# A three-stage attention and MLP kernel: splits, sums and loads of its last two stages put in another order

## The reference, cut to what matters

```python
attn = attention(q, k, v)                     # batch 4, 8 heads, 576 tokens, 64 wide; two window masks
xk = mu_k * x + (1 - mu_k) * x_prev           # x is attn as [4, 576, 512], x_prev is x one token back
xr = mu_r * x + (1 - mu_r) * x_prev
x = sigmoid(xr @ w_r) * (relu(xk @ w_k) ** 2 @ w_v)
h = relu(x.transpose(0, 2, 1) @ w_tok1) @ w_tok2      # over tokens: 576 -> 256 -> 576
u = x + h.transpose(0, 2, 1)
out = u + relu(u @ w_ch1) @ w_ch2                     # over channels: 512 -> 1536 -> 512
```

## Time and profile before

| | us |
|---|---|
| median of 3 runs | 744.74 |
| range of the runs | 740.33 to 745.08 |
| the profiled execution | 743.76 |
| its span in the profile | 741.9 |
| TensorE busy (matmul) | 672.7, 91% of the span |
| VectorE, ScalarE, GpSimd busy | 493.7, 320.2, 260.3 |

### The profile page before, as it was taken

How to read it: one execution, slowest core, us unless ns; L and a number is a source line. 1 busy time by engine, 2 the same in 40 slices (tenths; PEclk the granted TensorE clock), 3 DMA queues, 4 the chain that set the end, 5 groups by cost and what they waited for, 6 DMA issues and landing times.

```text
span 741.9 us, 17173 instructions
## 1 busy us (share of the span) xinstructions
PE 672.7 (91%) x6977; PEld 647.4 (87%) x6977; DVE 493.7 (67%) x836; ACT 320.2 (43%) x676; POOL 260.3 (35%) x289
## 2 busy tenths in 40 slices
PE   8999999999999999994898788999697639999997
PEld 7879999999999999993787788999697639989997
DVE  5588876766777676782476767767386336574855
ACT  4573645354444534541442255636264224142530
POOL 5575746464646464611863411120301300000000
PEclk9999999999999999998899979999898959999999
DMA  9962433324323316229671343546786494969783
GB/s 192 252 140 51 79 66 55 63 54 88 61 55 62 75 38 127 79 63 177 144 262 65 125 164 123 189 145 217 237 266 228 151 373 166 232 258 243 240 236 65
DMA packets 210174, 109.46 MB, mean 148 GB/s; under 512 B 163112, under 2 KB 199088, under 8 KB 209584
## 3 DMA queue, kind: packets, MB, share of 16 engines
q1 hardware_dynamic: 200144, 103.06, 50.1%
q10 hardware_dynamic: 9952, 5.31, 3.0%
HBM read 69.41 MB, written 38.93 MB: 146 GB/s over the span
## 4 chain that ended last, share of the span: by engine, by line
PE 68%; DMA 10%; DVE 9%; SPq 6%; ACT 2%; POOL 2%; issue 2%; POOLq 0%; DVEq 0%
PE bank L961 8%; PE bank L963 7%; PE bank L962 7%; PE tq L961 3%; DMA ck__raw<-h_rows 3%; SPq L1835 3%; PE tq L962 3%; PE tq L963 3%; PE bank L837 2%; DMA W__raw<-in_moe_w_ch 2%; PE bank L1556 2%; PE bank L1016 2%; PE bank L1558 2%; PE bank L1557 2%; PE s L625 2%; PE tq L1556 2%
## 5 line engine op out<-in xcount | busy, mean ns | idle before, releaser
L1744 ACT ACTIVATE ck__hi<-ck__raw 128x576 fp32r<-128x576 f32 x84 | 51.4, 674 | 85.3 <-DMA ck__raw<-h_rows 85.3
L1748 DVE TENSOR_TENSOR ck__lo<-ck__raw,ck__hi 128x576 fp32r<-128x576 f32 x84 | 58.9, 747 | 37.8 <-ACT ck__hi L1744 37.8
L1556 PE MATMUL bank<-U__hi,W__hi 128*128 128x288 f32 x192 | 59.8, 312 | 17.9 <-ACT hq L1592 11.9
L1056 POOL TENSOR_TENSOR k_lo<-kr,k_hi 128x288 fp32r<-128x288 f32 x64 | 56.2, 882 | 25.4 <-ACT k_hi L1052 25.4
L1098 DVE RECIPROCAL rg<-rg 128x288 f32<-128x288 f32 x32 | 61.4, 1922 | 0.0
L1557 PE MATMUL bank<-U__hi,W__lo 128*128 128x288 f32 x192 | 58.8, 306 | 0.0
L1558 PE MATMUL bank<-U__lo,W__hi 128*128 128x288 f32 x192 | 58.5, 305 | 0.0
L961 PE MATMUL bank<-k_hi,WV_hi 128*128 128x288 f32 x184 | 55.5, 301 | 0.0
L1556 PEld LDWEIGHTS bank<-U__hi,W__hi 128*128 128x128 f32 x192 | 38.1, 199 | 19.1 <-ACT hq L1592 12.4
L962 PE MATMUL bank<-k_hi,WV_lo 128*128 128x288 f32 x184 | 54.3, 295 | 0.0
L963 PE MATMUL bank<-k_lo,WV_hi 128*128 128x288 f32 x184 | 54.1, 294 | 0.0
(11 more groups left out here) (253 smaller groups left out, 2341.2 us busy)
## 6 DMA issues: line engine op xcount, KB each, us to landing
h_rows<-hq SPq DMA_DIRECT2D x24, 1008.0 KB, 4.6
ck__raw<-h_rows SPq DMA_DIRECT2D x28, 864.0 KB, 5.5
W__raw<-in_moe_w_ch SPq DMA_DIRECT2D x7, 768.0 KB, 7.9
x_turned<-xblocks SPq DMA_DIRECT2D x16, 288.0 KB, 5.2
u_kept<-X SPq DMA_DIRECT2D x4, 1152.0 KB, 8.8
ub<-u_kept SPq DMA_DIRECT2D x4, 1152.0 KB, 6.9
xT_raw<-x_turned SPq DMA_DIRECT2D x4, 1024.0 KB, 5.8
out_x<-ob SPq DMA_DIRECT2D x56, 72.0 KB, 3.4
```

The costliest lines, as they stand in the source:

```text
L1056: e.tensor_tensor(lo, t, hi.bitcast(F32), ALU.subtract).then_inc(Z.lo_done, 1)
L1556: e.matmul(ps, wh[:, w], xh[:, x], start=not onto and kt == 0, stop=False, skip_group_check=onto)
L1744: e.activation(hi, raw, ACT.Copy).then_inc(Z.ch_done, 1)
L1748: e.tensor_tensor(lo, raw, hi.bitcast(F32), ALU.subtract).then_inc(Z.cl_done, 1)
```

## The change

It touches the last three lists of steps, the places of some tiles and a few semaphores; the arithmetic is the same.

- `x_blocks(1)` goes three units earlier in `phase1`. `x_rows` is cut in `x_out` (store) and `x_in` (read back), placed apart; batch 3's blocks get a place of their own (that of batch 1's), so they no longer wait for batch 2's store.
- In the token stage `x_blocks(2)`, `x_blocks(3)` and the w1 sums come first, `token_up(b, 0)` goes ahead of `x_parts(b + 1)`, `token_up(b, 1)` behind it, and splits are moved.
- The sums are cut in single steps (`w1_sum`, `u_sum`, `w2_sum`). Those of w1 slice 2, of u for batches 2 and 3, and S1 and S2 of w2 go from GpSimd to VectorE.
- `u_parts` splits in the order in which TensorE uses the parts, and each half product waits for its own operand's split, not for all seven.
- `load_w2` has four parts, of which the first two come behind steps 7 and 11 (before: step 15). `w2_parts` for A12, S3, S4 and A22 come after the up stage's last step. `W2`, `CK`, `ub` and `ob` lie elsewhere, so that `load_h(2)` and `load_h(3)` can come behind step 22.

```diff
-        W2, o = [], 0
-        for i in range(7):
-            if i == 3:
-                o = R0
-            w, o = weights(f"W2_{i}_", [P, NJ * 2 * P], o)
-            W2.append(w)
-        a11_again = at("a11_again", [P, NJ * 2 * P], F32, R0 + 8 * NJ * 2 * P)
+        W2_AT = [0, 8 * NJ * 2 * P, 16 * NJ * 2 * P, R0, R0 + 8 * NJ * 2 * P, U1, U1 + 8 * NJ * 2 * P]
+        W2 = [weights(f"W2_{i}_", [P, NJ * 2 * P], off)[0] for i, off in enumerate(W2_AT)]
+        a22_first, a11_again = [at(n, [P, NJ * 2 * P], F32, W2_AT[i]) for n, i in (("a22_first", 1), ("a11_again", 4))]
+        NCK = 4
+        CK_AT = [U0, U0 + 8 * NJ * HALF, R0 + NSL1, R0 + NSL1 + 8 * NJ * HALF]
+        CK = [weights(f"ck{i}_", [P, NJ * HALF], off)[0] for i, off in enumerate(CK_AT)]
+        o = R0 + 2 * NSL1
         ub = [at(f"ub{i}", [P, DT * S], F32, o + 4 * DT * S * i) for i in range(2)]
-        o += 8 * DT * S
-        ob = at("ob", [P, DT * S], F32, o)
-        o += 4 * DT * S
-        NCK = 4
-        CK = [weights(f"ck{i}_", [P, NJ * HALF], (U0, U1)[i // 2] + 8 * NJ * HALF * (i % 2))[0] for i in range(NCK)]
-        assert o <= U0 and U0 + 16 * NJ * HALF <= U1 and U1 + 16 * NJ * HALF <= HQ0
+        ob = at("ob", [P, DT * S], F32, o + 8 * DT * S)
+        assert CK_AT[3] + 8 * NJ * HALF <= o and o + 12 * DT * S <= U0 and W2_AT[2] + 8 * NJ * 2 * P <= R0 - 4 * P - 16 * DT
...
-        xblocks = (xblocks0, xblocks1, xblocks2, xblocks2)
+        xblocks = (xblocks0, xblocks1, xblocks2, xblocks3)
...
+        def w1_sum(s, k):
             raw = [w[2][:, :] for w in W1[s]]
...
+            made, first = (Z.w1_last_sums, 0) if s == NSL - 1 else (Z.w1_sums, 4 * s)
+            def queue(e):
+                if k == 0:
+                    e.wait_ge(w1_in[s], 64)
+                    e.tensor_tensor(raw[S1], raw[S3], raw[A22], ALU.add).then_inc(made, 1)
+                elif k == 1:
+                    e.wait_ge(made, first + 1)
+                    e.tensor_tensor(raw[S2], raw[S1], raw[A11], ALU.subtract).then_inc(made, 1)
+                elif k == 2:
+                    e.wait_ge(made, first + 1)
+                    e.tensor_tensor(raw[S3], raw[A11], raw[S3], ALU.subtract).then_inc(made, 1)
+                else:
+                    e.wait_ge(made, first + 2)
+                    e.tensor_tensor(raw[S4], raw[A12], raw[S2], ALU.subtract).then_inc(made, 1)
+            return dict(vector=queue) if s == NSL - 1 else dict(gpsimd=queue)
...
-        U_ORDER = (B11, T1_, B21, B22, T3_, T2_, T4_)
+            def queue(e):
...
+            return dict(gpsimd=queue) if b < 2 else dict(vector=queue)
...
+                if j_ == 0:
+                    e.wait_ge(Z.ul_done, 7 * b_ + U_ORDER.index(i) + 1)
+                if b_ == 0 and j_ % 2 == 0:
+                    e.wait_ge(Z.w1_lo, 7 * (j_ // 2) + i + 1)
...
                 if part == 0:
                     e.wait_ge(Z.u_kept, 16 * B)
+                    e.wait_ge(Z.ul_done, 7 * 2)
+                    e.dma_start(tiles(W2[A11][2][:, :], NJ), w2_block(0, 0)).then_inc(Z.w2_in0, 16)
+                elif part == 1:
+                    e.wait_ge(Z.ul_done, 7 * 3)
+                    e.dma_start(tiles(W2[S1][2][:, :], NJ), w2_block(1, 0)).then_inc(Z.w2_in1, 16)
+                    e.dma_start(tiles(a22_first[:, :], NJ), w2_block(1, 1)).then_inc(Z.w2_in1, 16)
+                elif part == 2:
+                    e.wait_ge(Z.p4_done, NQ - 4)
+                    e.dma_start(tiles(W2[A12][2][:, :], NJ), w2_block(0, 1)).then_inc(Z.w2_in2, 16)
+                    e.dma_start(tiles(W2[S3][2][:, :], NJ), w2_block(1, 0)).then_inc(Z.w2_in2, 16)
+                    e.dma_start(tiles(a11_again[:, :], NJ), w2_block(0, 0)).then_inc(Z.w2_in2, 16)
+                else:
+                    e.wait_ge(Z.p4_done, NQ)
+                    e.dma_start(tiles(W2[S4][2][:, :], NJ), w2_block(0, 1)).then_inc(Z.w2_in3, 16)
+                    e.dma_start(tiles(W2[A22][2][:, :], NJ), w2_block(1, 1)).then_inc(Z.w2_in3, 16)
+            return dict(sync=sync)
...
+            def vector(e):
+                if i == S1:
+                    e.wait_ge(Z.w2_in1, 32)
+                    e.tensor_tensor(raw[S1], raw[S1], a22_first[:, :], ALU.add).then_inc(Z.w2_sums, 1)
+                else:
+                    e.wait_ge(Z.w2_in0, 16)
+                    e.wait_ge(Z.w2_sums, 1)
                     e.wait_ge(Z.ul_done, 7 * B)
...
+                    e.tensor_tensor(raw[S2], raw[S1], raw[A11], ALU.subtract).then_inc(Z.w2_sums, 1)
+            def gpsimd(e):
+                if i == S3:
+                    e.wait_ge(Z.w2_in2, 48)
+                    e.tensor_tensor(raw[S3], a11_again[:, :], raw[S3], ALU.subtract).then_inc(Z.w2_last_sums, 1)
                 else:
...
+                    e.wait_ge(Z.w2_in3, 32)
                     e.wait_ge(Z.w2_lo, S2 + 1)
...
+                    e.tensor_tensor(raw[S4], raw[S4], W2[S2][0][:, :].bitcast(F32), ALU.subtract).then_inc(Z.w2_last_sums, 1)
+                    e.wait_ge(Z.w2_last_sums, 2)
+                    e.tensor_tensor(raw[S4], raw[S4], W2[S2][1][:, :].bitcast(F32), ALU.subtract).then_inc(Z.w2_last_sums, 1)
+            return dict(vector=vector) if i in (S1, S2) else dict(gpsimd=gpsimd)
...
-                    e.wait_ge(Z.p4_done, NQ)
+                    e.wait_ge(Z.p4_done, NQ - 2)
...
-                ff[d // 2 - 6].append(x_blocks(1, d))
-            ff[-31].append(x_rows(0))
-            ff[-4].append(x_rows(1))
+                ff[d // 2 - 9].append(x_blocks(1, d))
+            ff[-31] += [x_out(0), x_in(0)]
+            ff[-7].append(x_out(1))
+            ff[-1].append(x_in(1))
...
-            steps = [x_parts(1, i) for i in range(NTT)] + [x_blocks(2, d) for d in range(DT)] + [x_rows(2)]
-            steps += [token_up(0, m) for m in range(2)] + [w1_sums(0)] + [x_parts(2, i) for i in range(NTT)]
-            steps += his(w1[0]) + token_rows(0) + [x_blocks(3, d) for d in range(DT)] + [x_rows(3), keep_u(0), u_sums(0)]
-            steps += [token_up(1, m) for m in range(2)] + his(u0) + [x_parts(3, i) for i in range(NTT)]
-            steps += los(w1[0])[:3] + token_rows(1) + [load_w1(1), keep_u(1)] + los(w1[0])[3:] + [w1_sums(1)]
-            steps += [token_up(2, m) for m in range(2)] + los(u0)[:3] + token_rows(2) + [keep_u(2)] + los(u0)[3:]
-            steps += [token_up(3, m) for m in range(2)] + his(w1[1]) + los(w1[1])[:3] + token_rows(3)
-            steps += [load_w1(2), keep_u(3), w1_sums(2), u_sums(1)]
+            steps = [x_blocks(2, d) for d in range(DT)] + [x_out(2)] + [w1_sum(0, k) for k in range(4)]
+            steps += [x_blocks(3, d) for d in range(DT)] + [x_out(3), token_up(0, 0)] + [x_parts(1, i) for i in range(NTT)]
+            steps += [token_up(0, 1), x_in(2)] + his(w1[0]) + los(w1[0])[:3] + token_rows(0) + [x_in(3), keep_u(0)]
+            steps += [u_sum(0, k) for k in range(4)] + los(w1[0])[3:]
+            steps += [token_up(1, 0)] + [x_parts(2, i) for i in range(NTT)] + [token_up(1, 1), load_w1(1)] + his(u0)
+            steps += token_rows(1) + los(u0)[:4] + [keep_u(1)]
+            steps += [token_up(2, 0)] + [x_parts(3, i) for i in range(NTT)] + [token_up(2, 1)] + [w1_sum(1, k) for k in range(4)]
+            steps += los(u0)[4:] + token_rows(2) + [keep_u(2)] + his(w1[1]) + los(w1[1])[:4]
+            steps += [token_up(3, 0), token_up(3, 1)] + los(w1[1])[4:] + token_rows(3)
+            steps += [load_w1(2), keep_u(3)] + [u_sum(1, k) for k in range(4)]
...
-            extra[0] += [w1[1][i][1] for i in range(3, 7)]
-            extra[2] += [x for i in range(4) for x in w1[2][i]]
-            extra[3] += [x for i in range(4, 7) for x in w1[2][i]]
-            for m in range(7):
-                extra[4 + m // 4] += u_parts(1, m)
+            extra[0] += [w1_sum(2, k) for k in range(4)]
+            extra[1] += [x for i in range(3) for x in w1[2][i]]
+            extra[2] += [x for i in range(3, 7) for x in w1[2][i]]
+            extra[3] += [x for m in range(3) for x in u_parts(1, m)]
+            extra[4] += [x for m in range(3, 7) for x in u_parts(1, m)]
             for b in (2, 3):
-                extra[NJ * (b - 1)].append(u_sums(b))
+                first = NJ * (b - 1)
+                for k in range(4):
+                    extra[first + k // 2].append(u_sum(b, k))
                 for m in range(7):
-                    extra[NJ * (b - 1) + 1 + m // 3] += u_parts(b, m)
-            extra[15] += [load_w2(0)]
-            extra[16] += [w2_sums(0)]
+                    extra[first + 2 + m // 3] += u_parts(b, m)
+            extra[7].append(load_w2(0))
+            extra[11].append(load_w2(1))
+            extra[17].append(w2_sum(S1))
+            extra[18] += [w2_sum(S2), load_h(0), load_h(1)]
             for i in range(3):
-                extra[17 + i].append(w2_parts(i))
-            extra[18] += [load_h(0), load_h(1)]
-            extra[20] += [load_w2(1), w2_sums(1)] + [chunk_parts(g) for g in range(3)]
```

(13 more changed lines are left out.)

107 lines of the change are left out of this document (38 added, 69 removed).

## The result

The changed kernel took 698.17 us (median of 4 runs, 695.37 to 702.92) beside 744.9 of the kernel before (740.33 to 745.08), a ratio of 0.9393 with a 95% interval of 0.9321 to 0.9465: faster by 46.7 us. The forecast was 701.5, its range 691 to 715. The profiled execution took 695.62, its span is 693.8, so 48.1 us less span than before. That execution lies at the lower end of the four. Ratios leave out executions more than 1.5% above the fastest of their kernel, of which e12 had one; medians keep them. Batches are numbered from 0 as in the code, and so are steps and chunks; what is "lost at chunk n" is a wait before its first matmul or slow matmuls behind it.

What follows compares the result with a forecast made beforehand. TensorE, busy 91% of the span, was taken as the bound, losing time in few long waits. Gains of 2.5 (token stage), 28.0 (up stage) and 11.9 (handover), 42.4 us off 743.76, gave 701.5; range 691 to 715.

Steps and rivals of the forecast that it cites:

- a wait of 4.5 instead of 10.1: Token stage, batch 0: TensorE's wait for h_lo, behind ScalarE's wait for batch 1's rows, shrinks from 10.1 to 4.5 us.
- the 1.7 I charge for a wait: Whole kernel: each TensorE wait above about 2.3 us costs 1.7 us more through the slower clock.
- if a batch of the token stage waits for rows longer than 6 us: Token stage: a sign that the forecast is wrong, a batch waiting over 6 us for its rows.
- 2.35 for steps 1 to 6: Early up steps: with sums moved to VectorE, TensorE loses 2.35 us in steps 1 to 6, against 15.1.
- 8.6 us gone: Up step 18: w2 loads issued earlier and sums standing long after landing remove its whole 8.6 us loss.
- a loss of 3.1, and 0.8 for the clock: Step 23, before the last up product: GpSimd's S3 sum holds VectorE's chunk splits, losing 3.1 us plus 0.8.
- 8.0: Handover to the down stage: losses around chunks 6 to 12 fall from 19.9 to 8.0 us, a gain of 11.9.
- the 12 that I had set as a sign of being wrong: Handover: the forecast is wrong if u(0) lands more than 12 us after the last product.
- A: Handover rival: transfers share bandwidth instead of coming in issue order, all ending near 568; total 712; chance 0.17.
- B: Rival: GpSimd and VectorE miss each other, S3's and S4's sums hold nothing; 3.9 and 4 us saved, total 694; chance 0.20.
- C: Token-stage rival: the stage gives nothing or costs 2 us, as a store takes longer; total 705; chance 0.10.
- D: Up-stage rival: VectorE becomes the bound with slow T operations, and the handover gains nothing; total 760; chance 0.03.

Runs made afterwards that it cites:

- e12: Changed kernel with the token stage reordered (VectorE's splits singly between the adds), plus e11's order of transfers: 694.65 us.
- e1: Changed kernel with the sums of w1 slice 2 and of u for batches 2 and 3 back on GpSimd: 704.67 us.
- e2: Changed kernel with the first two w_ch2 loads back behind step 15 and A12's split back behind step 21: 709.34 us.
- e5: Changed kernel with w2's S3 and S4 sums on VectorE, S3 behind step 24 and S4 behind chunk 8: 702.19 us.
- e13: e12 with S4's two subtractions, ahead of chunk 12's split, and batch 1's u sums, behind steps 1 and 2, on VectorE: 686.43 us.
- e4: Changed kernel with a batch's x splits, and VectorE's splits of w_ch1 and u, put behind rows in the token stage: 702.95 us.
- e6: Changed kernel with only S3's sum moved to VectorE, behind the last up step; S4's stays on GpSimd: 699.24 us.
- e7: Changed kernel with load_u(0) ahead of the last h_rows store and A12's w_ch2 block loaded one step later: 698.3 us.
- e11: e7's order of transfers on the changed kernel, with load_u(1) also moved behind load_h(4) and load_h(5): 700.71 us.
- e3: Changed kernel with w2's S1 and S2 sums on GpSimd and h loads of chunks 6 to 11 back behind step 24: 709.33 us.

## Why the prediction was right, and where it was off

**The bound.** TensorE's waits were the right ledger: the three stages and the start gave 48.1 us and the forecast had 42.4, with the up and down stages within 2 us each. The stages' sizes are right; several of the terms inside are not, and they cancel in part.

**Token stage: 2.5 forecast, 5.5 measured, from errors that partly cancel.** The mechanism of the first wait holds (ScalarE's `h_hi` behind `x_parts(1)`); the term "a wait of 4.5 instead of 10.1" was mis-sized (its own times, 342.3 + 1.2 to 348.4, make 4.9). The wait was 6.4; in this execution the read-back took 8.6 us and not 7.0, and where it took 7.1, in e1, e2 and e5, the wait was 5.0 to 5.2. The larger error is the clock after it, which cost far more than the 1.7 I charge for a wait: with clock 0.79 over 24.67 us, 10.4 us ran at 1.2 GHz. So the batch gained 0.2 and not 4.5. My own sign of being wrong, "if a batch of the token stage waits for rows longer than 6 us", came here: ScalarE waited 6.36 us for them and TensorE 6.4 behind it. In batch 1 I had TensorE wait from 364.1 to 367.5 for `h_lo`; there was nearly none, for batch 0 ended 3.6 us later than I said and the rows were there: what one wait costs the next one saves. Batch 2's wait for the adds was 3.1 where I said some 4, but its row has clock 1.00, so the 1.7 on top did not come. That is luck of one execution: the same program began the up stage 68.6 to 72.9 us after batch 0 in the nine profiles, and the 72.45 of the forecast lies within that.

**Up stage: 28.0 forecast, 29.8 measured.** Steps 13, 18 and 22 at 5.6 us, and "2.35 for steps 1 to 6" was 1.1. The rows of after and e13 give the price that no row of before had: a 128x512 sum on VectorE takes 0.69 (I took 0.7), and S4's 1536-column sums 1.76 (I took 1.75 for S1's and S2's). The reason that I gave for the early steps was too narrow. I tied the 15.1 us to the slow T operations beside GpSimd; with the sums back there (e1) T operations take up to 1.72 us and the steps lose 2.67. The splits' places carry the larger part (before's waits for `W__lo` and `U__lo`, e1, e4). In the same way "8.6 us gone" in step 18 has the right size and only part of its cause: late loads alone bring back 2.5 and GpSimd's sums alone 1.3; the working did not name the split that ScalarE stood at for 9.4 us, nor that the change puts it two steps later, and no run puts a price on that.

**Step 23: "a loss of 3.1, and 0.8 for the clock"; measured 3.25, without a slower clock.** The hold is as forecast, but a second wait came with it: ScalarE's copy behind a store that `load_w2(2)` delays. e5 and e6 show that without the hold 2.2 us stay.

**The handover: "8.0" lost, measured 5.8.** Chunk 6 waits 2.2 and chunk 12 1.7 us, and the clock is lower once for 3.4 us. `load_u(0)` is issued 5.2 us sooner than the 551.8 of the forecast, in a stage that began 5.6 sooner: as forecast. It landed at 554.6, 11.4 us after the last product's end, inside the 12 that I had set as a sign of being wrong. I had chunks 10, 11 and 12 lose 4.55 to S4's sums; it was 1.9. The hold is there, but TensorE reached the place late: e7 and e11, without the wait at chunk 6, lose 5.8 and 7.1 at chunks 12 to 14. That S4's chain held the last store is read from the two traces: it is issued 14.2 us into the down stage before (593.48) and 2.9 us into it now (546.15). Only the loads of h were put back by a run (e3, 4.4 us); S4's split was not. The rest was to stay at 8.3 and was 10.3: the loss at chunks 33 and 34 rose by 1.8.

**The rivals.** A (the transfers share) is wrong: `load_u(0)` landed 8.0 us after its issue, not 16. B (the two engines miss each other) is half right for S4. C and D did not come: T operations stayed at 460 ns with the longer VectorE queue. That 81 to 83% of VectorE can be filled without a loss is what D doubted.

## What to carry to other kernels

Where one engine is the bound and its waits are few, cost a reordering wait by wait, and then ask of each wait removed which one stood beside it or follows it: here batch 1's wait vanished because batch 0's stayed, step 23 had two waits on one chain, and a load moved forward made TensorE meet a hold that it had missed. An operation moved to an idle engine pays twice if it stops the busy one (GpSimd's sum of 3.5 us cost VectorE 3.2), and the same operation cost next to nothing on the busy engine at a place where that one waited for a load (e13). Read a change of order stage by stage: executions of one program differed here by 4 us in a stage that no edit touched.

## What the runs showed of the hardware

**The clock's price is not fixed to the wait's length.** In after a wait of 6.4 us was followed by about 10 us at 1.2 GHz, and a wait of 3.1 in batch 2 by none (clock 1.00 in its row). In e13 a wait of 3.1 us ahead of batch 2 was followed by 0.27 x 18.79 x 2 = 10.1 us at 1.2 GHz, so that this batch took 18.79 us where batch 3 took 13.15. A wait of 5.0 us in batch 0 was followed by 10.4 us at 1.2 GHz in e1 (clock 0.78 over 23.54 us) and by 3.5 in e2 (0.92 over 21.61). A charge of 1.7 us for each wait stands for outcomes that went from 0 to 5, and executions of one program differ by this.

**A VectorE operation with both inputs in SBUF stands still for a whole GpSimd operation**, also when GpSimd's begins less than 0.2 us before it: 3.94 us for 0.75 of work beside 3.46, and 5.28 for 1.5 across two sums. Between two sums 0.1 us apart one split did get its turn, and the second sum took 3.81 us instead of 3.5 for it.
